# POOL makes a slot's q/k difference and first weight block ahead of the g lo part of the slot's second step

## The reference, cut to what matters

```python
scores = scale * np.matmul(q, k.transpose(0, 1, 3, 2))
kth = np.partition(scores, -top_k, axis=-1)[..., -top_k:-top_k + 1]   # top_k = 32
scores = np.where(scores >= kth, scores, -1000000000.0)
attn = softmax(scores)                  # written out with max, exp, sum + 1e-09
x = np.matmul(attn, v)                  # heads put side by side: 2304 x 512
h = x @ w_in                            # layer 1, 512 -> 2048
g = np.where(h >= 1, h, np.where(h <= -1, 0.0, (h + 1) ** 2 / 4))
x = g @ w_out
h = np.maximum(x @ w2_in, 0.0)          # layer 2
out = (h * h) @ w2_out
```

## Time and profile before

| what | value |
|---|---|
| median of 3 runs | 1286.64 us (1285.8 to 1288.35) |
| the profiled execution, its own time | 1287.39 us |
| its span, first to last instruction | 1285.6 us |
| PE busy (matmul) | 1194.8 us, 93% |
| DVE busy | 910.6 us, 71% |
| POOL busy | 783.9 us, 61% |
| ACT busy | 721.8 us, 56% |
| mean granted TensorE clock | 0.975 of full |
| kq_lo on POOL (L1029) | 15 of 2849 ns |
| weight blocks on POOL (L1037), w_out and w_in | 15 of 2705 ns, 9 of 2364 ns |
| g_lo on POOL (L1063) | 288 of 754 ns |
| mask comparison on POOL (L1045) | 144 of 1794 ns |

### The profile page before, as it was taken

How to read it: one execution, slowest core, us unless ns; L and a number is a source line. 1 busy time by engine, 2 the same in 40 slices (tenths; PEclk the granted TensorE clock), 3 DMA queues, 4 the chain that set the end, 5 groups by cost and what they waited for, 6 DMA issues and landing times.

```text
span 1285.6 us, 24517 instructions
## 1 busy us (share of the span) xinstructions
PE 1194.8 (93%) x8760; PEld 1132.5 (88%) x8760; DVE 910.6 (71%) x2039; ACT 721.8 (56%) x1617; POOL 783.9 (61%) x637
## 2 busy tenths in 40 slices
PE   2677888999999999999999999999999999999998
PEld 1566878988888999999999999999989999999997
DVE  5789899989899998989999999989861111111121
ACT  4555566766655476776767654556543565643332
POOL 2999787787788776777766767666562222222222
PEclk9966799999999999999999999999999999999999
DMA  5899748565879972543437851445429500780000
GB/s 194 275 341 349 255 164 274 187 232 209 321 254 341 387 300 74 170 166 122 130 114 263 314 197 39 140 151 198 147 77 354 217 34 1 265 325 8 27 17 17
DMA packets 98728, 245.89 MB, mean 191 GB/s; under 512 B 7344, under 2 KB 48304, under 8 KB 86320
## 3 DMA queue, kind: packets, MB, share of 16 engines
q1 hardware_dynamic: 98608, 244.33, 53.7%
HBM read 167.23 MB, written 77.07 MB: 190 GB/s over the span
## 4 chain that ended last, share of the span: by engine, by line
PE 69%; POOL 11%; ACT 8%; DVE 5%; issue 4%; DMA 1%; SPq 0%; ACTq 0%; POOLq 0%
PE h_ps L581 21%; PE y_ps L602 14%; PE y_ps L596 12%; PE pv_ps L540 6%; PE score_ps L581 6%; POOL s_sb L1045 4%; PE tr_ps L513 4%; POOL prob L1050 3%; PE score_ps L478 3%; DVE top L860 2%; DVE rest L862 2%; ACT prob L699 1%; POOL kq_lo L1029 1%; POOL w_out L1037 1%; ACT s_sb L676 1%
## 5 line engine op out<-in xcount | busy, mean ns | idle before, releaser
L1063 POOL TENSOR_TENSOR g_lo<-g_sb,g_hi 128x256 fp32r<-128x256 f32 x288 | 217.2, 754 | 405.1 <-ACT g_hi L778 404.9
L581 PE MATMUL h_ps<-xt_hi,w_in 128*128 128x256 f32 x1880 | 391.3, 291 | 3.5 <-DVE xt_lo L908 2.0
L581 PEld LDWEIGHTS h_ps<-xt_hi,w_in 128*128 128x128 f32 x1880 | 309.6, 191 | 6.7 <-issue 3.0
L860 DVE MAX8 top<-rest 128x8 f32<-128x576 f32 x432 | 303.8, 744 | 0.0
L1045 POOL TENSOR_SCALAR s_sb<-s_sb,top 128x576 f32<-128x576 f32 x144 | 258.4, 1794 | 51.5 <-DVE top L860 50.6
L581 PE MATMUL h_ps<-xt_lo,w_in 128*128 128x256 f32 x940 | 266.2, 283 | 0.0
L596 PE MATMUL y_ps<-g_hi,w_out 128*128 128x256 f32 x1152 | 232.6, 285 | 0.4 <-POOL g_lo L1063 0.3
L778 ACT ACTIVATE g_hi<-g_sb 128x256 fp32r<-128x256 f32 x288 | 121.0, 420 | 184.7 <-DVE g_sb L917 68.8
L862 DVE MATCH_REPLACE8 rest<-top,rest 128x576 f32<-128x576 f32 x288 | 211.4, 741 | 0.0
L602 PE MATMUL y_ps<-w_out,g_hi 128*128 128x512 f32 x576 | 203.3, 394 | 0.3 <-POOL g_lo L1063 0.3
L596 PEld LDWEIGHTS y_ps<-g_hi,w_out 128*128 128x128 f32 x1152 | 190.4, 193 | 1.7 <-POOL g_lo L1063 0.5
(11 more groups left out here) (79 smaller groups left out, 1954.9 us busy)
## 6 DMA issues: line engine op xcount, KB each, us to landing
w_in<-w_scratch SPq DMA_DIRECT2D x32, 1024.0 KB, 6.7
w_out<-w_scratch SPq DMA_DIRECT2D x32, 1024.0 KB, 8.0
ks<-ks_scratch SPq DMA_DIRECT2D x47, 576.0 KB, 5.5
qs<-qs_scratch SPq DMA_DIRECT2D x78, 256.0 KB, 4.4
stage<-in_w_dram SPq DMA_DIRECT2D x32, 512.0 KB, 4.7
w_scratch<-w_in SPq DMA_DIRECT2D x16, 1024.0 KB, 6.8
w_scratch<-w_out SPq DMA_DIRECT2D x16, 1024.0 KB, 8.3
v_sb<-in_vv_dram SPq DMA_DIRECT2D x48, 325.0 KB, 5.5
```

The lines of the kernel that those rows point to most:

```text
L581: last = pe.matmul(h_bank(k), wi[:, f // 2, w, m, cols], x[:, m, :], start=(m == 0 and n == 0), stop=(m == KT - 1 and n == 2))
L860: dve.max(best, src[:, :]).then_inc(rank_step, 1)
L1063: pool.tensor_tensor(g_lo[k % 2][:, :], g_sb[k % 2][:, :], g_hi[k % 2][:, :].bitcast(F32), ALU.subtract).then_inc(g_lo_done, 1)
```

## The change

In the function that lists POOL's slot, the kq_lo of the slot and the first weight block that POOL makes in it are put between g_lo of position 3n and g_lo of position 3n + 1. A second weight block of the slot stays behind. The test for DVE's blocks moves from split_w to the list. No instruction is added, removed or changed in shape, and no wait is changed; those on other engines keep their order.

```diff
             def split_w(i):
-                if by_vector(i):
-                    return
                 pool.wait_ge(w_hi_done, i + 1)
                 b = w_block(i % WBLOCKS)
...
                 if before:
                     mask(n - 1, 1)
                 lo_at(q)
-                lo_at(q + 1)
+                new = [i for i in range(2 * WBLOCKS) if W_SLOT[i] == n and not by_vector(i)]
                 if n in PREP_SLOT:
                     split_kq(PREP_SLOT.index(n))
-                for i in range(2 * WBLOCKS):
-                    if W_SLOT[i] == n:
-                        split_w(i)
+                for i in new[:1]:
+                    split_w(i)
+                lo_at(q + 1)
+                for i in new[1:]:
+                    split_w(i)
```

## The result

The changed kernel takes 1300.2 us (median of 4 runs, 1298.38 to 1302.49) against 1287.5 us before (4 runs): a ratio of 1.0098, 95% interval 1.0078 to 1.0117. That is 12.7 us slower, where +14.2 was forecast.

What follows compares the result with a forecast made beforehand. The loop of mask, ACT, DVE's g_sb and rank was taken to bound slots 11 to 28. Terms -0.2 + 4.3 + 7.7 + 1.1 + 0 + 1.3 = +14.2 us gave 1300.8 us, range 1288 to 1309.

Steps and rivals of the forecast that it cites:

- What bounds the kernel: Slots 11 to 28: time runs round mask, ACT, DVE's g_sb, rank, mask; PE waits 18.6 us for the masked prob.
- What it gives: Moved instruction no longer stands ahead of the mask: 0.96 us less in kq_lo slots where rank isn't later, nothing in 20.
- The rival case: Gain shows and the meeting doesn't hold DVE up: 6.9 us less over the slots, 1279.7 us; chance 0.13.
- What it costs: Second-step g_sb waits for the moved POOL instruction's end, delaying rank and mask: mask +0.98 us in slot 13, +0.95 in 20.
- d: Delay of second-step g_sb: moved instruction's start plus length, less g_sb's start, less 0.15 us.
- The sum by stretch: Slots 10, 11: -0.2 us; 12 to 17: +4.3; 19 to 28: +7.7; 30, 32: +1.1; 38 to 47: 0; clock +1.3.
- The clock: Longer PE waits, 1.38 to about 2.4 us, may lower PE's granted clock: +1.3 us, bounds 0 and 4 times 1.3.
- Costed at nothing: Later second-step g_lo, SP's writes some 3 us earlier, and DVE's later arrival in slot 14: no cost.
- The rule weighed: Skill's rule of whole-length holding against rows where g_sb beside TENSOR_SCALAR lost only 0.19 us; the sum follows the row.
- Signs named: Slots 12 to 26: g_sb 1.8 to 2.4 us, mask 0.2 behind rank; prob waits some 30; stretch after 700 us unchanged.

Runs made afterwards that it cites:

- the kernel that waits in some slots: Changed kernel, POOL also waiting for second-step g_sb before the moved instruction, but old order in slots 20 to 24 and 26 to 28: 1280.1 us, ratio 0.9953.
- The last kernel: Against the kernel that waits in some slots: POOL's block in 20, 21, 23, 24, 26, 27 moved too, behind g_sb, in halves: 1276.2 us.
- the kernel that waits: Changed kernel, with POOL also waiting for DVE's second-step g_sb ahead of the moved instruction in all 21 slots: 1282.3 us, ratio 0.9966.
- The one-input runs: The 21 subtractions replaced by products with zero: 1291.3 us in changed order, 1296.8 in old, 1277.7 in changed order with kq_lo cut into 1024 and 192.
- the kernel with all in halves: Changed kernel with each of the 21 moved subtractions cut into two of half the columns: 1287.0 us, ratio 1.0003.

## Why the prediction was right

The direction, the mechanism and the size were right; 12.7 us measured, 14.2 forecast. Step by step:

- *What bounds the kernel.* Right. The loop of mask, ACT, g_sb and rank sets the time of slots 11 to 28: with g_sb at 0.42 us in the same order the kernel is 17 us faster, and the mask starts 0.2 us behind rank in every kernel whose POOL work fits ahead of it. But the loop doesn't end at slot 28: of the 7.5 us that the kernel that waits in some slots gains in its profile, 4.0 lie in slots 30 to 48, where PE was read as nearly always finding its input ready.
- *What it gives.* Right, and a little under-priced. The rival case has 6.9 us for the 21 slots, 6.0 of them in the 14 slots without a block on DVE; the kernel that makes the move in these 14 alone, behind g_sb, gained 6.6 us. Slots 30 and 32, which the rival case left out, gave 0.6 us each. The last kernel gained 11.5 us; it also takes the meeting away from DVE's weight blocks (1.21 in place of 1.69 us), a gain that the rival case didn't count.
- *What it costs.* Right. Slot 13: d = 1.94 forecast, 2.50 - 0.43 = 2.07 measured; slot 20: 1.40 and 1.46, with -0.45 and -0.49 on DVE's block; slot 38: 0.78 and 0.82. In nine of the eleven slots from 12 to 26 with a moved instruction g_sb took 1.43 to 2.50 us; in 23 it was the pair of xt_lo that was held (3.45 us for the two, 1.29 before) and in 25 nothing.
- *The sum by stretch*, from PE's times_v in the profile: slots 10 to 18 +6.4 (forecast 4.1 and part of the clock), slots 19 to 29 +6.2 (7.7; the terms named for these slots add to 7.45), slots 30 to 33 -0.4 (+1.1), slots 38 to 48 0.0 (0). The first is itself a sum of -1.6 in slots 10 and 11 (-0.2 forecast) and +8.0 in slots 12 to 18 (4.3). The -1.6 is mostly a shorter stretch at the lower clock (granted 0.57, 0.50 and 0.79 before in the three stretches from 141 to 150 us, 0.78, 0.66 and 1.00 in the changed kernel), and that varies with the execution: two profiles of the kernel that waits in some slots stand 0.1 us behind and 2.5 us ahead of the kernel before at slot 11. So the total is as near as it is partly by luck: more was lost in slots 12 to 18 than forecast, and less in 10, 11 and from 19 on. The mis-sized term from 19 on is that of slots 28 and 30, where g_sb and the end of the first g_lo are 0.1 us apart or less. In 28 kq_lo came first and g_sb took 3.10 us (0.6 us was charged, 1.6 measured); in 30 g_sb came first, took 0.43 and the slot gained 0.6 (bounds 0 to 2.5 for 30 and 32 together; -0.4 lies outside them).

```profile
390.21 2.82 POOL L1029 TENSOR_TENSOR kq_lo<-kq_lo,kq_hi 128x1216 fp32r<-128x1216 f32 x1
...
390.21 3.10 DVE L923 TENSOR_TENSOR g_sb<-r_sb 128x256 f32<-128x256 f32 x1 [0.73 <-ACT r_sb L764]
...
418.44 3.01 POOL L1029 TENSOR_TENSOR kq_lo<-kq_lo,kq_hi 128x1216 fp32r<-128x1216 f32 x1
...
418.34 0.43 DVE L923 TENSOR_TENSOR g_sb<-r_sb 128x256 f32<-128x256 f32 x1 [0.63 <-ACT r_sb L764]
```

- *The clock.* Taken at 1.3 us. PE's waits of 1.4 us became up to 2.6, and slots 15, 17 and 20 are followed by stretches at a lower granted clock (the column before the last two; 0.50 is the level of 1.2 GHz), while the kernel before had one such stretch in slots 12 to 28, from 318 to 324 us (0.66 and 0.77). Waits of 2.3 and 2.6 us in slots 13 and 14 of the changed kernel were followed by none:

```profile
213.00:216.00 3.00, 2.09 (x12) 2.12 (x13) 3.00 (x10) 2.41 (x5) 2.92 (x3) 0.72 1.05 395
...
240.00:243.00 3.00, 2.19 (x12) 2.02 (x13) 2.85 (x7) 2.18 (x4) 2.92 (x2) 0.77 0.80 329
...
283.00:286.00 3.00, 3.00 (x16) 3.00 (x15) 3.00 (x10) 2.66 (x5) 2.92 (x3) 0.50 1.01 427
```

  PE's busy time rose from 1194.8 to 1197.8 us for the same instructions, though slots 10 and 11 had less of the low clock, so the term is rather too small; no run separates it.
- *Costed at nothing.* Right: g_lo of the second step came 3.6 us behind g_sb in the kernel that waits, and cost nothing. That DVE's later g_sb of the next slot comes behind the mask's product was right too: 1.23 us before, 0.41 at 188.38. Of SP's earlier work only half was right. ACT's wait of 1.96 us in slot 25 for a weight block from DRAM is gone in the changed kernel: in SP's program the load waits until the block but one before it is split, and that is earlier now. Six of the thirteen profiles have the old order in slot 24, and ACT waits 1.89 to 3.25 us in all of them; of the seven with the moved order six have 0.25 us or nothing, and the last kernel, whose ACT comes there earlier, has 2.14. It was worth nothing where PE had slack, but in two other executions, with the lower clock that came behind it, it cost 2 to 3 us.
- *The rule weighed.* The rows were kept over the rule for the mask comparison, rightly: g_sb of the third step still takes 0.61 us beside it. The one-input runs show what lay behind the difference: a one-input instruction holds g_sb too, but up to 1024 columns only for its first 0.7 to 1.0 us.
- *Signs named.* The held g_sb took 1.43 to 2.50 us, not 1.8 to 2.4, and two of the eleven weren't held; PE's waits for prob reached 25.1 us and not 30; the stretch after 700 us grew by the 0.8 us of the DMA wait. That the held g_sb end 0.28 us behind POOL's instruction, and the mask 0.2 us behind rank's, came as named.

## What to carry to other kernels

Filling an engine's idle time is only free if what is put there doesn't shut out the engine whose result that idle time was waiting for: here POOL idled for DVE's g_sb, and the subtraction put there held g_sb up for its whole length. Before moving a two-input POOL instruction, look at which two-input DVE instruction comes due in its new place, and put it behind that one with a wait, or cut it so that DVE gets in between. On an engine pair with such a meeting the later start can be the faster one: one added wait per slot turned 1300 us into 1282.

## What the runs showed of the hardware that was not expected

- A one-input POOL instruction (TENSOR_SCALAR, f32) beside a two-input DVE instruction: with 576 columns g_sb ended 1.02 us behind its start, with 1024 columns 1.31 us, with 1216 columns 3.22 us, of durations of 1.73, 2.79 and 3.29 us. Less the 0.28 us of g_sb itself DVE was held 0.74, 1.03 and 2.94 us. So it is held for the first part of the instruction up to 1024 columns and nearly to its end with 1216; cut into 1024 and 192 the 1216 columns hold it 1.04 us. Where between 1024 and 1216 it turns, and why, stays open. With two inputs DVE was held to the end at 256, 512, 608, 1024 and 1216 columns.
- It works both ways. A POOL subtraction that comes due while DVE's weight block runs waits for it: both halves took 3.51 us with DVE's 1.21 us between them, and 2.56 us in slot 25 of the kernel with all in halves, where no two-input DVE instruction came between.
